# Routing each batch as it is made: rows scattered into one region per expert, first 16 blocks from two batches, last batch routed inside the expert stage

## The reference

```python
X = np.fft.fft(x, axis=1); X = np.fft.fft(X, axis=2); x = X.real
logits = xn @ en.T / tau                 # xn, en: rows by their norms
expert_idx = np.argmax(logits, axis=1)
gate_w = softmax(logits)[np.arange(N), expert_idx]
for e in range(E):                       # 8 experts, D 256, F 1024
    mask = expert_idx == e
    h = np.maximum(x[mask] @ w1[e], 0.0)
    out[mask] = gate_w[mask, None] * (h @ w2[e])
# channel mix: xk, xr from x and the row before it
k = np.maximum(xk @ w_k, 0.0); out = sigmoid(xr @ w_r) * (k * k @ w_v)
```

## Time and profile before

| | us |
|---|---|
| median of 3 runs | 1606.61 |
| lowest, highest | 1606.55, 1608.92 |
| time of the profiled execution | 1606.98 |
| its span, first to last instruction | 1605.1 |
| PE busy | 1505.6 |
| DVE busy | 1035.9 |
| ACT busy | 896.1 |
| POOL busy | 340.2 |

### The profile page before, as it was taken

One profiled execution on the slowest core, in us unless ns is written; L12 is line 12 of the kernel. 1 busy time (PEld: TensorE's weight loads), 2 busy tenths in 40 slices (PEclk: granted clock), 3 DMA queues, 4 the chain that ended last, 5 costly groups with the idle time before them and its releaser, 6 DMA issues.

```text
span 1605.1 us, 30457 instructions
## 1 busy us (share of the span) xinstructions
PE 1505.6 (94%) x11046; PEld 1435.8 (89%) x11046; DVE 1035.9 (65%) x1665; ACT 896.1 (56%) x1709; POOL 340.2 (21%) x375
## 2 busy tenths in 40 slices
PE   6988856699999999999999978999999999999998
PEld 6878736699999999999999977999999999999998
DVE  4766679666666566666666636767676666767574
ACT  1553436476566566665665635656565555556563
POOL 2331227373333333333333310000000000000000
PEclk9998977799999999999999998999999999999999
DMA  8054211665565665665655510110101010101010
GB/s 230 1 158 144 93 79 54 247 241 214 206 234 197 209 240 198 223 224 199 230 216 199 221 39 29 38 52 27 52 26 52 26 52 26 52 26 52 26 40 27
DMA packets 56248, 196.84 MB, mean 123 GB/s; under 512 B 13942, under 2 KB 40326, under 8 KB 46984
## 3 DMA queue, kind: packets, MB, share of 16 engines
q1 hardware_dynamic: 45640, 171.02, 30.5%
...
...
## 4 chain that ended last, share of the span: by engine, by line
PE 88%; DVE 5%; issue 3%; POOL 1%; DMA 1%; ACT 1%; SPq 0%; DVEq 0%; POOLq 0%; ACTq 0%
PE ps L603 77%; PE ps L531 3%; PE ps L562 2%; PE ps L611 2%; PE ps L660 1%; PE ps L551 1%; DVE hot_blk L1058 1%; PE ps L552 1%; DVE zv L979 1%; DMA xg<-rows,idx 0%; ACT d L729 0%; DMA tau_b<-tau 0%; DVE cum L1018 0%; ACT square L757 0%; DVE k2f L1151 0%
## 5 line engine op out<-in xcount | busy, mean ns | idle before, releaser
L603 PE MATMUL ps<-we,ht 128*128 128x256 f32 x2640 | 329.7, 284 | 0.0
L603 PE MATMUL ps<-xgt,we 128*128 128x256 f32 x2640 | 327.8, 284 | 1.4 <-DVE xgt L1087 1.4
L603 PEld LDWEIGHTS ps<-xgt,we 128*128 128x128 f32 x2640 | 322.7, 193 | 1.8 <-DVE xgt L1087 1.8
L603 PEld LDWEIGHTS ps<-we,ht 128*128 128x128 f32 x2640 | 319.8, 192 | 0.0
L1098 DVE SCALAR_TENSOR_TENSOR ht<-ps,ht 128x512 fp32r<-128x512 f32 x220 | 146.2, 684 | 217.4 <-ACT ht L789 217.2
L603 PE MATMUL ps<-w_split,k_split 128*128 128x256 f32 x2304 | 280.5, 283 | 0.2 <-DVE k_split L1144 0.2
L603 PEld LDWEIGHTS ps<-w_split,k_split 128*128 128x128 f32 x2304 | 278.2, 192 | 0.4 <-DVE k_split L1144 0.4
L603 PE MATMUL ps<-x_split,w_split 128*128 128x512 f32 x1152 | 268.0, 392 | 6.1 <-DVE x_split L1139 6.1
L1093 DVE TENSOR_TENSOR we<-we_raw,we 128x1024 fp32r<-128x1024 f32 x220 | 263.3, 1218 | 13.5 <-ACT we L779 13.4
L603 PEld LDWEIGHTS ps<-x_split,w_split 128*128 128x128 f32 x1152 | 216.1, 189 | 50.7 <-DVE x_split L1139 6.5
L859 ACT ACTIVATE relu<-ps 128x512 f32<-128x512 f32 x192 | 115.0, 599 | 214.8 <-PE ps L603 214.8
...
## 6 DMA issues: line engine op xcount, KB each, us to landing
...
xg<-rows,idx POOLq DMA_INDIRECT x110, 4.8
moe<-yo,idx_out POOLq DMA_INDIRECT x110, 5.2
...
```

Of the source, the lines that this page charges most:

```text
L603: ins = mm(o, a(i), b_(k), start=first_ and n == 0, stop=last_ and n == 2)
```

## The change

`rows` now holds one region of `CAPR` rows for each expert, and a row carries two numbers behind its 256 values, its gate and its number in the result. As soon as a batch has its choices, a running count per expert (`run`) gives each row its place; POOL scatters the batch's 24 slots there, one indirect DMA of 128 rows for each slot. For batches 0 to 2 this happens in the next batch: DVE works out the places at `st` 1 (`within`) and 4 (`place`), PE the counts at `st` 2 (`rank`, two matmuls of 8 columns), POOL scatters 6 slots among its `xr` operations and 18 behind `rinv`. From the counts of batches 0 and 1 DVE makes the table of the first 16 blocks (`early_table`). Block 0's weights and rows are loaded during batch 3, block 0's rows are transposed in its step 11, and its first weights are split by ACT in its step 13. The last batch's routing runs in blocks 0 to 5, its scatters in blocks 5 to 7 (8 each), and blocks 16 to 54 take their places from a second table. A block is then a contiguous piece of a region, loaded by SP with a plain DMA, and `ids` gives POOL the rows for the result. The index lists and their 96 tables are gone. `xr` has three buffers, the first half of a batch uses three pairs of PSUM banks, the four batches and the first 17 blocks are written out, and the channel mix's weights are split in blocks 12 to 14.

```diff
-ROW = D + 1
+ROW = D + 2
...
-MBP = 112
+NE = 16
+NL = NB - NE
+LEAD = 17
+XB = (0, 1, 2, 0)
+RES_AT, RES_PER = (5, 6, 7), 8
+IN_FFT = 6
...
-C_SPLIT_AT = (1, 2, 3)
-R_EXP, R_STEPS = 7, 14
+WORK = 49400
+C_SPLIT_AT = (12, 13, 14)
...
+        def d_bank(c):
+            return 2 * (c % 3)
...
+            def load_rows(i, s):
+                r = sp.value_load(row_of[0:1, bass.ds(i, 1)], min_val=0, max_val=E * CAPR)
+                sp.dma_start(xg[s].rearrange("p j c -> p (j c)"),
+                             rows[bass.ds(r, BT), :].rearrange("(p j) c -> p (j c)", j=HB)).then_inc(gathered[s], 16)
...
+            sp.wait_ge(d_early, 1)
+            for n in range(2):
+                sp.wait_ge(pair_ready[n], use("f1", NC - 2 + n, B - 1) + 1)
+            load_w(1, 1)
+            for b in range(2):
+                sp.wait_ge(rows_out[b], 16 * N2)
+            e = sp.value_load(expert_of[0:1, 0:1], min_val=0, max_val=E - 1)
+            sp.dma_start(we_first[:], w_e[bass.ds(e, 1)].rearrange("o p c -> p (o c)")
+                         ).then_inc(w_first, 16)
+            for n in range(2):
+                sp.wait_ge(z_done[n], B * (NC // 2))
+            load_rows(0, 0)
+            load_rows(1, 1)
+            load_w(2, 0)
...
+            def load_tails():
+                sp.wait_ge(d_late, 1)
+                for e in range(E):
+                    r = sp.value_load(tail_at[0:1, e:e + 1], min_val=0, max_val=E * CAPR)
+                    sp.dma_start(rows[bass.ds(r, BT), :].rearrange("(p j) c -> p (j c)", j=HB),
+                                 tailc.rearrange("p j c -> p (j c)")).then_inc(d_tail, 16)
+            def m_step(i, s):
+                sp.wait_ge(m_meta, i + 1)
+                if not isinstance(i, int) or i + 2 < NB:
+                    load_rows(i + 2, s)
+                if not isinstance(i, int) or i + 3 < NB:
+                    sp.wait_ge(w_low, (i + 2) * WP)
+                    load_w(i + 3, 1 - s)
...
+            def rank(b):
+                pe.wait_ge(r_step, (b + 1) * R_STEPS + R_EXP + R_CHOICE)
+                pe.wait_ge(d_tab, 16 * 3)
+                wait(pe, p_step, (b - 1) * P_STEPS + P_SCAN + 2)
+                mm(ps[:, 7, 0:E], before[:], rowsum[:], start=True, stop=True)
+                mm(ps[:, 7, E:2 * E], ones[:], rowsum[:], start=True, stop=True).then_inc(d_rank, 1)
...
                     if c < 2:
                         pe.wait_ge(ab_ready[c], ab_count(NK - 1 - c, b - 1))
+                    elif c == 2:
+                        pe.wait_ge(eo_ready, b * NK + PRIME)
                     else:
-                        pe.wait_ge(z_done[c % 2], b * (NC // 2) + c // 2)
+                        pe.wait_ge(z_done[(c - 3) % 2], b * (NC // 2) + (c - 3) // 2 + 1)
                     for g in range(GC):
                         for dc in range(DC):
...
+                    if b and st == 2:
+                        rank(b - 1)
+                    if b == B - 1 and st == NK - 2:
+                        rows_in(0, 0)
...
+                if isinstance(i, int) and i == 2:
+                    rank(B - 1)
                 down(i, s)
...
-                    copy(d0[c % 2], ps[:, 2 * (c % 2), 0:GC * KP]).then_inc(d0_ready, 1)
-                    if c == 5:
-                        before_(act, b, q, bb, exponential)
+                    if c >= 2:
+                        act.wait_ge(z_done[c % 2], b * (NC // 2) + c // 2)
+                    copy(d0[c % 2], ps[:, d_bank(c), 0:GC * KP]).then_inc(d0_ready, 1)
+                    if b and c == 5:
+                        exponential(b - 1)
...
+                    if b == B - 1 and st == NK:
+                        act.wait_ge(w_first, 16)
+                        w_high_first(0)
+                        w_high_first(1)
+                        rows_a(0)
...
+            w_high_first(2)
+            w_high_first(3)
...
+                link(v.tensor_tensor(onehot[:], iota_t, over_e(pick), ALU.is_equal))
+                link(v.tensor_reduce(rowsum[:], onehot.rearrange("p t e -> p e t"), AX.X, ALU.add), wait_now=False)
...
+            def within(b):
+                link = chain(p_step, b * P_STEPS)
+                dve.wait_ge(r_step, (b + 1) * R_STEPS + R_EXP + R_CHOICE)
+                link(copy(scan[0][:, :, 17:16 + N2], onehot[:, 0:N2 - 1, :].rearrange("p t e -> p e t")))
+                a, z = scan
+                for sh in (1, 2, 4, 8, 16):
+                    link(v.tensor_tensor(z[:, :, 16:16 + N2], a[:, :, 16:16 + N2], a[:, :, 16 - sh:16 + N2 - sh],
+                                         ALU.add))
+                    a, z = z, a
+                assert link.n[0] == P_SCAN
+            def place(b):
+                link = chain(p_step, b * P_STEPS + P_SCAN)
+                dve.wait_ge(d_rank, b + 1)
+                link(v.tensor_tensor(rbase[:], run[:], ps[:, 7, 0:E], ALU.add))
+                link(v.tensor_tensor(run[:], run[:], ps[:, 7, E:2 * E], ALU.add))
+                link(v.tensor_tensor(place3[:], scan[1][:, :, 16:16 + N2],
+                                     rbase[:].unsqueeze(2).to_broadcast([P, E, N2]), ALU.add))
+                link(v.tensor_tensor(place3[:], place3[:], onehot.rearrange("p t e -> p e t"), ALU.mult))
+                link(v.tensor_reduce(posf[:], place3.rearrange("p e t -> p t e"), AX.X, ALU.add))
+                assert link.n[0] == P_STEPS - P_SCAN
+                copy(pos[:, b * N2:(b + 1) * N2], posf[:]).then_inc(pos_ready, 1)
...
+            def early_table():
+                dve.wait_ge(p_step, P_STEPS + P_SCAN + 2)
+                t_link(v.scalar_tensor_tensor(cnt[:], iota_e[0:1, :], -float(CAPR), run[0:1, :], ALU.mult, ALU.add))
+                t_link(v.tensor_scalar(quot8[:], cnt[:], 1.0 / BT, -0.5 * (BT - 1) / BT, ALU.mult, ALU.add))
+                t_link(copy(full[:], quot8[:]))
+                at_ = running(full, E - 1)
+                t_link(v.tensor_scalar(delta[:, 0:E - 1], full[:, 0:E - 1], -float(BT), float(CAPR), ALU.mult, ALU.add))
+                t_link(v.tensor_scalar(used[:], at_, -1.0, float(NE), ALU.mult, ALU.add))
+                t_link(v.scalar_tensor_tensor(used[:], used[:], 0.0, full[:], ALU.max, ALU.min))
+                table(0, NE, at_[:, 1:E], E - 1, None)
+                copy(row_of[:, 0:NE], where[:, 0:NE]).then_inc(d_early, 1)
...
+                    if b and st == 1:
+                        within(b - 1)
...
+                        if k2 == 0 and b == B - 1:
+                            dve.wait_ge(rows_out[0], 16 * N2)
...
+                    if b and st == 4:
+                        place(b - 1)
+                    if b == 2 and st == 8:
+                        early_table()
+            w_low_first(0)
+            w_low_first(1)
+            rows_v(0, 0)
+            w_low_first(2)
+            w_low_first(3)
...
+            def meta(i, s):
+                dve.wait_ge(gathered[s], 16 * (i // 2 + 1))
                 wait(dve, m_y, i - 1)
-                copy(gates[s][:], xg[s][:, :, D:ROW].rearrange("p j o -> p (j o)")).then_inc(m_gate, 1)
-                dve.wait_ge(m_xh, i + 1)
-                v.tensor_tensor(xgt[:, 1, :, :].rearrange("p c t -> p (c t)"), ps[:, 6, :],
-                                xgt[:, 0, :, :].rearrange("p c t -> p (c t)").bitcast(F32), ALU.subtract).then_inc(m_xt, 1)
+                wait(dve, scattered[s], i // 2 * (16 * HB))
+                copy(gates[s][:], xg[s][:, :, D:D + 1].rearrange("p j o -> p (j o)"))
+                copy(ids[s][:], xg[s][:, :, D + 1:ROW].rearrange("p j o -> p (j o)")).then_inc(m_meta, 1)
...
+                if isinstance(i, int):
+                    if i == 0:
+                        scores(B - 1)
+                    if i == 1:
+                        choice(B - 1)
+                    if i == 2:
+                        gate(B - 1)
+                        within(B - 1)
+                    if i == 3:
+                        place(B - 1)
+                    if i == 4:
+                        late_counts()
+                    if i == 5:
+                        late_table()
+            pairs(dve, LEAD, NB, m_step)
...
+            def scatter_rows(b, t0, t1):
+                if t0 == 0:
+                    pool.wait_ge(gate_done, b + 1)
+                    pool.wait_ge(pos_ready, b + 1)
+                for t in range(t0, t1):
+                    g.indirect_dma_start(out=rows, in_=xr[XB[b]][:, SLOTS[t], :], in_offset=None,
+                                         out_offset=bass.IndirectOffsetOnAxis(ap=pos[:, b * N2 + t:b * N2 + t + 1], axis=0),
+                                         bounds_check=last_row, oob_is_err=False).then_inc(rows_out[b], 16)
+            for b in range(B):
+                xo = xr[XB[b]]
                 for k2 in range(1, NK - 1):
                     pool.wait_ge(eo_ready, b * NK + k2 + 1 + PRIME)
-                    if k2 == 1:
-                        pool.wait_ge(xr_free[q], bb + PRIME)
```

(24 more changed lines are left out.)

524 lines of the change are left out of this document (226 added, 298 removed).

## The result

The changed kernel takes 1564.43 us in the median of four runs (1557.67 to 1565.76), the kernel before beside it 1607.28: a ratio of 0.9724, interval 0.9701 to 0.9747. The profiled run took 1563.33 us with a span of 1561.5; the forecast was 1550, its range 1533 to 1577. On two further chips of the same kind the unedited kernel gave 0.9704 (0.9685 to 0.9723; 1559.28 us) and 0.9942 (0.9921 to 0.9963; 1594.4 us), while the kernel before took 1606.4 and 1606.2 there. The second of these is out of the range, and half of what follows is about it.

What follows compares the result with a forecast made beforehand. PE, never idle in the expert stage, was taken as the bound, leaving gains only between stages, chiefly the 77.53 us routing hole. Terms -72.6 - 12.2 + 10.9 + 6.9 + 0.6 + 9.8 = -56.6 us gave 1550 us, range 1533 to 1577.

Steps and rivals of the forecast that it cites:

- Term 1: Between last transform and block 0: common routing goes, 77.53 us replaced by a hand-over of about 4.9; -72.6 us.
- Term 2: First halves of the FFT: loop turn 7.9 us and third bank pair 4.3 us saved; -12.2 us.
- Terms 3 to 5: In the FFT: DVE's new work in second halves +10.9, POOL's scatters +6.9, block 0's transposes in batch 3 +0.6 us.
- `place` is directly ahead of the `ab` copy at step 5: Second halves: `place` takes 1.8 us on DVE against slack of 0.38, so 1.4 us reach PE.
- term 4: POOL's scatters in the FFT, inside steps and behind `rinv`: +6.9 us, at the least 2, at the most 25.
- slower: Rival: long bursts of indirect DMAs at 1.87 + 0.30 us an issue, 96 on the path; 1618 us, chance 0.04.
- full blocking: Rival: DVE's operations fully block POOL's issues, in FFT steps and early blocks; 1574 us, chance 0.17.
- Term 6: POOL and DVE in the first blocks: block 2 loses 8.3 us, 1.5 us more by block 8; +9.8 us.
- some 6 us of room after a landing: Block 8: POOL about 9 us behind, DVE's copies have some 6 us of room; costs 1.5 us.
- queued behind them: Block 2: hidden 1 to 3 and low weights queue on DVE behind copies awaiting a scatter's landing; PE loses 8.3 us.
- the steady block stays: Expert stage: the steady block keeps its length of 11.95 us.
- Blocks from 9 on at 11.95: Sign in the expert stage: every block from 9 on takes the steady 11.95 us.

Runs made afterwards that it cites:

- done alone: Kernel before with only the four batches written out and three PSUM bank pairs, no scatters in the transform: 1593.6 us against 1606.19, ratio 0.9915.
- the odd steps: Changed kernel with DVE's `place` moved from step 4 to 5 and the block table from step 8 to 9: 1587.04 us, 7.4 below the unedited kernel.
- the first and third edit: Against the changed kernel: block's scatter ahead of `w_split`'s low part in blocks 12 to 14, 1578.16 us; DVE's `gates` copy behind the next block's rows, 1563.72 us.
- the first session: First measurement of the unedited changed kernel, beside the kernel before: 1564.43 us, ratio 0.9724.
- chip 1: Chip of the second session of the unedited changed kernel: 1594.4 us, ratio 0.9942 to the kernel before.

## Why the prediction came out where it did

**Term 1, -72.6.** Measured 77.53 - 4.99 = 72.5. The rows and weights of block 0 were in time, as taken: no wait of PE stands ahead of its transposes.

**Term 2, -12.2.** In the profile the four first halves are 0.7, 2.1, 10.0 and 2.0 us shorter, 14.9 in all; done alone it gave 12.6. The term holds. The third pair is under-sized (1.1 us a batch, 2.0 and 2.1 in batches 3 and 1), and not by the waits: in batch 1 PE's idle time is 5.0 us before and after, and what falls is its busy time, from 16.84 to 14.67 us at a mean granted clock of 0.91 and 0.97. With `zv` no longer awaited in between, PE's one long stop is at the end.

**Terms 3 to 5, +18.4.** The second halves are 0.6, 3.9, 9.9 and 5.7 us longer: 20.1. The step "`place` is directly ahead of the `ab` copy at step 5" is what the odd steps confirmed; for the table they do not show it. In term 4 the parts were mixed up: scatters inside the steps cost 0.1 us in batch 1, not 2. What the end of the burst of 18 costs was not isolated; only that a further 7.7 us of it cost 5.4 to 6.6. The "at the most 25" of that term was too low by my own figures: the rival "slower" has 54 issues in the transform at 0.85 us more, 46 us.

**The lock that I argued away.** I set the median of the earlier trace rows, 1.02 us with DVE busy 65% of a block, against the rival "full blocking". That was a wrong reading: what counts is which operation runs as an issue begins. In the kernel before, 58 of the 220 indirect DMAs begin under a subtraction of weights, and all 58 take 1.20 to 2.05 us; in the changed one it is 19 of 206, as shown above. The Trainium skill ("SBUF — State Buffer", SBUF: two separate sides) calls the port pair that DVE and GpSimd share an exclusive lock, held for the whole instruction by whichever starts first, and counts DVE's operations with two inputs in SBUF among those that take it. The trace agrees in both directions, with 19 issues out of 19 and with DVE's 4.19 us, and the operations with an input in PSUM hold nobody up. So the mechanism of that rival is real and its price is not: in the steps of the transform no issue takes over 1.18 us, and the six long issues of the burst behind batch 3 cost POOL 3.5 us, where term 6 has 4 and the rival 10. That burst took 26.4 us, where I had 27.8.

Up to block 0 the sum was -66.4, measured -67.55.

**Term 6, +9.8; measured +24.7** (from block 0's first matmul to the end of the last block 683.7 us against 659.0). This is the step that failed, in three parts. Block 2 was right in mechanism and size: 7.4 us for 8.3, with a wait of 7.19 us (hidden 1 was due at 44.6 by its own terms, not 44.7). Blocks 5 to 8 were right in mechanism and too small: 6.4 us instead of 1.5; my "some 6 us of room after a landing" counted from the landings of the earlier trace rows, and in the changed kernel a result's scatter takes 5.8 us in the median and up to 8.7. Blocks 13 and 15 were not in the prediction: 15.5 us. The prediction's own rule, "queued behind them", was applied to POOL's scatters and not to POOL's low part of `w_split`, which is not new: the change only moves it to blocks 12 to 14. Before, nobody but ACT's `result` waited for the scatter behind it; the new copy in DVE made it critical, as the first and third edit show. Of block 13, one wait of 3.73 us is the lock. Against that, "the steady block stays" was wrong by 0.08 us a block, 4.6 us in 55 with block 0's share, in our favour; nothing was tried for its cause. Together 7.4 + 6.4 + 15.5 - 4.6 = 24.7, 14.9 more than the term. Less 1.1 before block 0 and 0.7 in the channel mix, that is the distance from 1550.4 to 1563.3.

**The ranges of the time.** That the time lies in the range owes something to luck twice: the unforeseen 15.5 us were partly made up by a steady block that was 4.6 faster than I took it, and the first session was one without late signals. The 1594 us of chip 1 have their cause outside every case of the prediction. The rival "slower, by long bursts" named the right object with the wrong mechanism: an issue there takes 0.98 us as well. What it costs, two halves longer by 14.5 and 14.9 us, less 5.5 in the second halves of batches 1 to 3 and 4.0 ahead of batch 1, is 20 us up to block 0, and the blocks are 9 longer (40 us over the steady pace instead of 31).

**What would show it.** First matmul at 226.61 (225 to 232), second halves 30.7 to 37 us (29 to 34, batch 2's outside), issues at 1.28 (1.3), DVE's wait in block 2 7.19 (6 to 11): these held. "Blocks from 9 on at 11.95" did not, and it was the signpost to the error. "Faster by over 0.2%" held in all three sessions in which the unedited kernel ran, if on chip 1 by 0.6% only.
